# One kernel, one edit: all score tiles of a head pair before its value products, in attention run beside a feed-forward layer

## What is computed

```python
scores = 1.0 / np.sqrt(64) * np.matmul(q, k.transpose(0, 1, 3, 2))
scores = cap * np.tanh(scores / cap)
scores = scores - np.max(scores, axis=-1, keepdims=True)
attn = np.exp(scores)
attn = attn / (np.sum(attn, axis=-1, keepdims=True) + 1e-09)
x = np.matmul(attn, v)                 # then (B*S, H*D) = (1792, 768)
r = np.maximum(x @ w_in, 0.0)
y = (s * (r * r) + b) @ w_out
```

## Time and profile before

| | us |
|---|---|
| median of three runs | 625.81 |
| lowest, highest | 625.52, 625.81 |
| the profiled execution's own time | 625.56 |
| its span, from first to last instruction | 623.8 |

### The profile page before, as it was taken

One profiled execution on the slowest core, in us unless ns is written; L12 is line 12 of the kernel. 1 busy time (PEld: TensorE's weight loads), 2 busy tenths in 40 slices (PEclk: granted clock), 3 DMA queues, 4 the chain that ended last, 5 costly groups with the idle time before them and its releaser, 6 DMA issues.

```text
span 623.8 us, 8172 instructions
## 1 busy us (share of the span) xinstructions
PE 617.9 (99%) x3206; PEld 480.8 (77%) x3206; DVE 331.4 (53%) x565; ACT 258.3 (41%) x272; POOL 46.0 (7%) x46
## 2 busy tenths in 40 slices
PE   8999999999999999999999999999999999999998
PEld 4335666777777777777779999999988888888998
DVE  5986999998677677677663332222411121111221
ACT  7985455656555555555413322222411121111220
POOL 0115724700000000000000000000000000000000
PEclk9999999999999999999999999999999999999999
DMA  8432245342222222221014111222522234111501
GB/s 293 139 118 61 87 155 158 107 132 92 73 92 87 76 88 91 71 92 58 29 60 145 62 51 55 73 73 80 172 78 59 68 106 130 48 38 31 171 2 64
DMA packets 31863, 57.17 MB, mean 92 GB/s; under 512 B 3536, under 2 KB 18000, under 8 KB 31824
## 3 DMA queue, kind: packets, MB, share of 16 engines
q1 hardware_dynamic: 31824, 56.64, 28.0%
HBM read 40.11 MB, written 16.52 MB: 91 GB/s over the span
## 4 chain that ended last, share of the span: by engine, by line
PE 96%; ACT 2%; DVE 1%; issue 1%; DVEq 0%; ACTq 0%
PE banks L480 13%; PE banks L482 13%; PE banks L481 13%; PE banks L493 12%; PE banks L492 12%; PE banks L494 12%; PE banks L438 8%; PE banks L393 5%; PE banks L352 3%; PE banks L450 2%; PE banks L418 1%; ACT e L636 1%; PE banks L461 1%; PE banks L509 0%; ACT e L623 0%
## 5 line engine op out<-in xcount | busy, mean ns | idle before, releaser
L480 PE MATMUL banks<-x_hi,w_hi 128*128 128x448 f32 x384 | 142.9, 372 | 0.0
L482 PE MATMUL banks<-x_hi,w_lo 128*128 128x448 f32 x384 | 140.7, 366 | 0.0
L481 PE MATMUL banks<-x_lo,w_hi 128*128 128x448 f32 x384 | 140.6, 366 | 0.0
L493 PE MATMUL banks<-x_lo,w_hi 128*128 128x512 f32 (+2 forms) x384 | 139.4, 363 | 0.0
L494 PE MATMUL banks<-x_hi,w_lo 128*128 128x512 f32 (+2 forms) x384 | 139.4, 363 | 0.0
L492 PE MATMUL banks<-x_hi,w_hi 128*128 128x512 f32 (+2 forms) x384 | 139.4, 363 | 0.0
L821 DVE SCALAR_TENSOR_TENSOR x_lo<-e,beside,x_hi 128x512 fp32r<-128x512 f32 (+1 forms) x48 | 32.5, 684 | 115.4 <-ACT x_hi L650 115.4
L480 PEld LDWEIGHTS banks<-x_hi,w_hi 128*128 128x128 f32 x384 | 72.1, 188 | 15.0 <-issue 8.3
L650 ACT ACTIVATE x_hi<-e,beside 128x512 fp32r<-128x512 f32 (+1 forms) x48 | 31.7, 669 | 116.7 <-PE banks L494 116.7
L492 PEld LDWEIGHTS banks<-x_hi,w_hi 128*128 128x128 f32 x384 | 72.1, 188 | 9.0
L493 PEld LDWEIGHTS banks<-x_lo,w_hi 128*128 128x128 f32 x384 | 72.1, 188 | 8.9
(11 more groups left out here) (67 smaller groups left out, 551.3 us busy)
## 6 DMA issues: line engine op xcount, KB each, us to landing
hidden_scratch<-hidden_sb SPq DMA_DIRECT2D x48, 224.0 KB, 1.9
beside<-q_k SPq DMA_DIRECT2D x23, 448.0 KB, 3.9
e<-hidden_scratch SPq DMA_DIRECT2D x32, 256.0 KB, 2.7
e<-w_out SPq DMA_DIRECT2D x16, 384.0 KB, 3.0
work<-w_in SPq DMA_DIRECT2D x22, 256.0 KB, 5.5
v_sb<-v SPq DMA_DIRECT2D x24, 192.0 KB, 2.5
y_t<-beside SPq DMA_DIRECT2D x10, 256.0 KB, 2.1
e<-hidden_scratch SPq DMA_DIRECT2D x16, 160.0 KB, 2.2
```

Source lines behind the costliest of these rows:

```text
L480: nc.tensor.matmul(out, w_hi[:, j, w], x_hi[:, batch % 2, c, :], start=c == 0, stop=False)
L481: nc.tensor.matmul(out, w_hi[:, j, w], x_lo[:, batch % 2, c, :], start=False, stop=False)
L482: last = nc.tensor.matmul(out, w_lo[:, j, w], x_hi[:, batch % 2, c, :], start=False, stop=c == CT - 1)
L493: nc.tensor.matmul(out, w_hi[:, j, w], ring(x_lo, n), start=False, stop=False)
```

## The change

1. In slots 6 to 22, tile 2 of pair p+1 (A2 B2) is computed right behind tiles 0 and 1, ahead of `values(p)`. It goes to the two `hid` banks. Two waits stand for that: `free_hidden` (before tile 2: the hidden tiles of the slot before have been rectified) and one in `hidden_chunk` (before the first hidden tile of a slot: `last_tanh` has read tile 2). The wait ahead of the next pair's scores is now on `first_read` and, for an odd pair, on the new semaphore `tails_read`.
2. The tail scores go to banks 2 and 3, and ACT reads them with a tanh of their own (`tails_tanh`), so an even pair has two instructions of 128x896 where it had one of 128x1792.
3. A slot's share is whole hidden tiles: 2, 2, 3, 2, 2, 3 in slots 6 to 11 and 3, 2, 3, 3, 2, 3 in each later batch (`tiles_beside`). The number of matmuls is the same.
4. On ACT `first_tanh` and `last_tanh` stand together at the front of the slot, and `split_high` behind them.
5. In `invert`, the copies to `quads` are sums over one element, and the reciprocal is taken four times, straight into `recips`, where one reciprocal and four copies stood.
6. On DVE the first tile of a slot is squared before `invert` and the others behind it.

The diff, with most of its context and two like hunks left out:

```diff
--- before.py
+++ after.py
@@ -33,10 +33,12 @@
 PIECES = CT * FF // PIECE
-CHUNKS = JT * CT
-SHARE = CHUNKS // PAIRS
-EARLY = 2 * CT
+EARLY = 2
+FIRST_ENDS = (4, 6, 9, 11, 13, 16)
+ENDS = (3, 5, 8, 11, 13, 16)
+assert len(ENDS) == len(FIRST_ENDS) == PAIRS and ENDS[-1] == FIRST_ENDS[-1] == JT
@@ -194,16 +197,19 @@
-        def chunks_of(batch, c):
-            if batch == 0:
-                share = (CHUNKS - EARLY) // PAIRS
-                return EARLY + share * c, EARLY + share * (c + 1)
-            return SHARE * c, SHARE * (c + 1)
-        def tiles_in(first, last):
-            return [j for j in range(JT) if first <= CT * j + CT - 1 < last]
+        def tails_group(p):
+            return (p - PAIRS) // 2
+        def tiles_beside(batch, c):
+            ends = FIRST_ENDS if batch == 0 else ENDS
+            first = EARLY if batch == 0 else 0
+            return range(ends[c - 1] if c else first, ends[c])
+        def first_tiles(batch):
+            return [tiles_beside(batch, c).start for c in range(PAIRS) if (batch + 1) * PAIRS + c + 1 < ALL] if batch < B - 1 else []
@@ -313,9 +319,9 @@
                 if p == PAIRS:
-                    for j in tiles_in(0, EARLY):
+                    for j in range(EARLY):
                         store_hidden(j)
-                for j in tiles_in(*chunks_of(batch - 1, c)):
+                for j in tiles_beside(batch - 1, c):
                     store_hidden((batch - 1) * JT + j)
@@ -352,6 +358,19 @@
+            def free_scores(p):
+                pe.wait_ge(first_read, first_group(p - 1))
+                if p == PAIRS + 1:
+                    pe.wait_ge(last_read, last_group(PAIRS))
+                elif p % 2:
+                    pe.wait_ge(tails_read, tails_group(p - 1))
+            def free_hidden(p):
+                batch, c = divmod(p - 1, PAIRS)
+                pe.wait_ge(relu_done, (batch - 1) * JT + tiles_beside(batch - 1, c).start)
             def first_scores(p):
@@ -360,7 +379,7 @@
-                if p > 0:
+                if 0 < p <= PAIRS:
                     pe.wait_ge(first_read, first_group(p - 1))
@@ -370,7 +389,7 @@
                 else:
-                    pe.wait_ge(last_read, last_group(p - 1))
+                    free_scores(p)
                     for t in range(FULL - 1):
@@ -470,6 +488,9 @@
                     pe.wait_ge(last_read, last_group(PAIRS - 1))
+                if c == 0 and j in first_tiles(batch):
+                    pe.wait_ge(last_read, last_group((batch + 1) * PAIRS + first_tiles(batch).index(j) + 1))
                 if batch == 0 and c == 0 and j % JPP == 0:
@@ -539,24 +560,24 @@
                 if p + 1 < SPLIT:
                     first_scores(p + 1)
+                    free_hidden(p + 1)
+                    last_scores(p + 1, G1)
                 elif p + 1 < ALL:
                     first_split_scores(p + 1)
+                    free_hidden(p + 1)
+                    last_split_scores(p + 1, G1)
                 values(p)
...
                     tail_values(p - 1, 2)
-                if p + 1 < ALL:
-                    pe.wait_ge(first_read, first_group(p + 1))
-                    if p % 2:
-                        tail_scores((p + 1) // 2, 0)
-                    bank = 2 if p % 2 else 0
-                    if p + 1 < SPLIT:
-                        last_scores(p + 1, bank)
-                    else:
-                        last_split_scores(p + 1, bank)
-                for chunk in range(*chunks_of(batch - 1, c)):
-                    hidden_chunk(batch - 1, chunk)
+                    if p + 1 < ALL:
+                        pe.wait_ge(first_read, first_group(p + 1))
+                        tail_scores((p + 1) // 2, 2)
+                for j in tiles_beside(batch - 1, c):
+                    for c_in in range(CT):
+                        hidden_chunk(batch - 1, CT * j + c_in)
@@ -604,6 +625,12 @@
                 act.wait_ge(last_done, p + 1)
+                if p > PAIRS:
+                    tile = tile_of(p, FULL - 1, 0)
+                    nc.scalar.activation(e[:, tile:tile + 2, :], hid[:, :, 0:S], ACT.Tanh, scale=tanh_scale
+                                         ).then_inc(last_read, 1)
+                    return
                 if p % 2 == 0:
@@ -619,8 +646,16 @@
                 else:
-                    source = banks[:, 0:2, 0:S] if p % 2 else banks[:, 0:4, 0:S]
+                    source = scores[:, :, 0:S]
                 nc.scalar.activation(e[:, group_of(p, 1), :], source, ACT.Tanh, scale=tanh_scale).then_inc(last_read, 1)
+            def tails_tanh(p):
+                act.wait_ge(tails_done, p // 2 + 1)
+                act.wait_ge(pv_done, products(p - 1))
+                act.wait_ge(e_sum_done, 3 * p)
+                nc.scalar.activation(e[:, G1:G1 + 2, :], scores[:, 2:G1, 0:S], ACT.Tanh, scale=tanh_scale
+                                     ).then_inc(tails_read, 1)
@@ -633,6 +668,8 @@
                 act.wait_ge(last_read if group else first_read, last_group(p) if group else first_group(p))
+                if group and p > PAIRS and p % 2 == 0:
+                    act.wait_ge(tails_read, tails_group(p))
                 nc.scalar.activation(e[:, group_of(p, group), :], e[:, group_of(p, group), :], ACT.Exp, scale=cap_c
@@ -667,20 +704,21 @@
                 exponential(p, 1)
-            for j in tiles_in(0, EARLY):
+            for j in range(EARLY):
                 rectify(j)
...
                 batch, c = divmod(p, PAIRS)
-                if SPLIT <= p + 2 < ALL:
-                    split_high(p + 2)
                 if p + 1 < ALL:
                     first_tanh(p + 1)
+                    last_tanh(p + 1)
+                    if SPLIT <= p + 2 < ALL:
+                        split_high(p + 2)
                     exponential(p + 1, 0)
-                if p + 1 < ALL:
-                    last_tanh(p + 1)
+                    if p % 2:
+                        tails_tanh(p + 1)
                     exponential(p + 1, 1)
-                for j in tiles_in(*chunks_of(batch - 1, c)):
+                for j in tiles_beside(batch - 1, c):
                     rectify((batch - 1) * JT + j)
@@ -760,18 +798,17 @@
                 for k in range(1, P // BLOCK):
-                    nc.vector.tensor_copy(quads[:, k, :], parts[k * BLOCK:(k + 1) * BLOCK, :]).then_inc(quads_done, 1)
+                    nc.vector.tensor_reduce(quads[:, k, :], parts[k * BLOCK:(k + 1) * BLOCK, :].unsqueeze(2), AX.X, ALU.add
+                                            ).then_inc(quads_done, 1)
                 dve.wait_ge(quads_done, P // BLOCK * (m + 1))
-                nc.vector.tensor_reduce(totals[:, 0, :], quads[:].rearrange("p k n -> p n k"), AX.X, ALU.add
+                nc.vector.tensor_reduce(totals[:], quads[:].rearrange("p k n -> p n k"), AX.X, ALU.add
                                         ).then_inc(totals_done, 1)
                 dve.wait_ge(totals_done, m + 1)
-                nc.vector.reciprocal(totals[:, 1, :], totals[:, 0, :]).then_inc(inverse_done, 1)
-                dve.wait_ge(inverse_done, 2 * PAIRS + m + 1)
...
                     head = k * BLOCK // D
-                    nc.vector.tensor_copy(recips[k * BLOCK:(k + 1) * BLOCK, 0, :],
-                                          totals[:, 1, head * BLOCKS:(head + 1) * BLOCKS]).then_inc(spread_done, 1)
+                    nc.vector.reciprocal(recips[k * BLOCK:(k + 1) * BLOCK, 0, :],
+                                         totals[:, head * BLOCKS:(head + 1) * BLOCKS]).then_inc(spread_done, 1)
                 dve.wait_ge(spread_done, P // BLOCK * (m + 1))
@@ -878,12 +915,11 @@
                     add_last_e(p + 1)
-                start, end = chunks_of(batch - 1, c)
-                for j in tiles_in(start, start + 8):
-                    square((batch - 1) * JT + j)
+                tiles = tiles_beside(batch - 1, c)
+                square((batch - 1) * JT + tiles[0])
                 if p + 1 < ALL:
                     invert(p + 1)
-                for j in tiles_in(start + 8, end):
+                for j in tiles[1:]:
                     square((batch - 1) * JT + j)
             for j in range(JT):
```

More of the change, by code:

```diff
@@ L92, in attention_ffn @@
         quads = sb("quads", [BLOCK, P // BLOCK, 2 * BLOCKS], F32)
-        totals = sb("totals", [BLOCK, 2, 2 * BLOCKS], F32)
+        totals = sb("totals", [BLOCK, 2 * BLOCKS], F32)
         r_sum = sb("r_sum", [P, 2, S], F32)
@@ L141, in attention_ffn @@
         last_read = sem("last_read")
+        tails_read = sem("tails_read")
         exp_done = sem("exp_done")
```

## The result

| | before | after |
|---|---|---|
| median, lowest to highest (six runs each, same chip), us | 625.66, 625.38 to 625.82 | 621.49, 621.08 to 621.78 |
| the profiled execution's own time, us | 625.56 | 621.75 |
| its span, us | 623.8 | 619.7 |

The ratio is 0.9934, 95% interval 0.9921 to 0.9947: 4.2 us faster, where 3.1 were foreseen (622.7, range 621.3 to 624.5).

What follows compares the result with a forecast made beforehand. TensorE's own work was taken as the bound. Joined score runs save 0.6 us (slots 6 to 8) plus 2.5 (9 to 22), 3.1 in all: 625.56 to 622.4, median 622.7 us; range 621.3 to 624.5.

Steps and rivals of the forecast that it cites:

- What bounds the kernel: TensorE, busy 99% of the span, waits for nobody from slot 6; only its own work or new waits move time.
- Edges, 3.1 us: Joining two score runs into one saves 0.20 us in each of slots 6 to 8, 0.18 in 9 to 22.
- The seam that is left: Hidden matmuls straight behind values (even slots) or tail scores (odd): no extra cost, values staying 2.41 us, tail scores 0.86.
- Rival (a): The seam moves and only half the edge is saved in 17 slots: 1.5 us, 624.3 us; chance 0.12.
- free_hidden: TensorE's new wait before tile 2 for the previous slot's last hidden tile to be rectified: margin 0.5 us, cost zero.
- Tile 2's tanh: First hidden tile waits until ACT has read tile 2: margin 0.12 us in seven even slots, 10 to 22.
- or the cast ahead of them: With the cast ahead of the two tanh on ACT, the margin of the first hidden tile's wait would be missed.
- worth nothing by itself: Cheaper invert saves DVE about 2 us beside POOL, but off the path, since TensorE doesn't wait for DVE.
- Whole tiles at zero: Shares of whole hidden tiles: same chunk count, some slots shorter, some longer, last slot ending at the same matmul; no gain counted.
- Rival (c): Late cast, DVE can't catch up in slots 8 to 11, late stores hold rectify and TensorE: 628.1 us; chance 0.05.
- rival (b): Hidden matmuls' pace changes: slots 12 to 22 faster, 620.8 us, chance 0.05; or slots 6 to 11 slower, 623.6, 0.03.
- the same pace as before: Sign that the forecast is right: hidden matmuls keep their pace, 0.203 us in slot 7 and 0.2065 in slot 14.

Runs made afterwards that it cites:

- seam_more: Changed kernel with tile 2 computed between the first and second value tiles, two more runs in each of 17 slots: 626.83 us, ratio 1.0015 to the kernel before.
- exp_between: Changed kernel with ACT's first exponential put between the tanh of tiles 0 and 1 and that of tile 2: 636.25 us, ratio 1.0172 to the kernel before.
- cast_first: Changed kernel with the cast of q and k (split_high) back at the front of ACT's slot: 621.06 us, ratio 0.9929 to the kernel before.
- old_invert: Changed kernel with the old copies back in invert: 622.05 us, ratio 0.9942 to the kernel before.
- whole_tiles: Kernel before with only the shares made whole hidden tiles, old invert kept: 629.7 us, ratio 1.0052 to the kernel before.
- cast_first_old_invert: Changed kernel with both the cast back at the front of ACT's slot and the old copies in invert: 624.08 us, ratio 0.9975 to the kernel before.

## Why the prediction was right

By its own steps:

- **What bounds the kernel**: held. TensorE has no wait from slot 6 on, and all of the gain is its own work.
- **Edges, 3.1 us**: measured 3.30. The 0.18 a run, read off rows in which two tiles and one tile stand apart, is also the mean of 34 further runs in seam_more.
- **The seam that is left, taken at zero**: held, 2.41 and 0.86 to the next start, now with hidden matmuls behind them. Rival (a), 624.3, falls.
- **`free_hidden`**: no wait in the kernel after. **Tile 2's tanh**: margin 0.2 for 0.12; the order of the two tanh is worth the 15 us that exp_between lost.
- **"or the cast ahead of them"** (it would be missed): wrong, and by the prediction's own numbers. It had the cast's end at T + 1.47 and `first_tanh`'s start at T + 1.53, so the cast fits ahead of it. cast_first shows it.
- **`invert` "worth nothing by itself"**: wrong. It was read from TensorE's waits before, where the slots were long enough. With the shorter whole-tile slots DVE is late in slots 9 to 11, and the new `invert` is what covers it: 1.45 us of the stretch in the one profiled execution of old_invert (0.6 of the median, not clear of noise), 3.2 us of the median in the order of before. The new `invert` in the kernel before, with its old shares, wasn't run. The 2 us per `invert` beside POOL was 2.8.
- **Whole tiles at zero**: it fits the sum only with the new `invert`; alone they were 4 us slower, and with the new `invert`, in the order of before, 0.9. Rival (c) had this chain, a late load, late DVE, stores on SP, but feared the cast's new place; that place covers the late load, and the danger lay in the shares with the old `invert`.
- **Pace**: rival (b), with 0.05 on the faster side, came in part: there are 330 slow matmuls fewer than 528, net 1.25 us of its 1.9. The forecast's sign "the same pace as before" didn't hold. This is the term that the sum left out and most of the surplus. The range left this rival's full size, 620.8, out. The measured 621.49 is 0.2 above the range's lower end because 330 matmuls changed and not 528, which nothing in the prediction foresaw; that part is luck.

The balance of the spans: 3.12 foreseen for the edges, + 0.18 there, + 1.25 of pace, - 0.51 of a late start that repeats of either kernel show to be chance, is 4.04 of 4.1.

## What to carry to other kernels

Where TensorE is the bound, count its runs of unlike tiles: each run here cost 0.15 to 0.20 us, and joining two gained that in each of 17 slots, since the wait for the bank was hidden by another run. When a step is called free since nobody waits for it, ask whether the same change shortens what covers it: take it out of the changed kernel, not only of the old one. And measure a kernel's repeated matmuls slot by slot, since equal ones may not be equally fast.

## What the hardware showed that I had not expected

Equal hidden matmuls (128 by 128, 448 columns, each with its weight load) keep one of two paces for a whole run of 36 to 54, 202.7 or 206.7 ns. The same slots were slow in both executions of the same kernel, with stretches equal to a nanosecond over 254 us. In kernels without a wait of TensorE in the stretch the choice follows the order and lengths of the runs ahead, and a new table of shares moved those at 206.7 ns from 360 to 36. A wait changes it: the same queue on TensorE had 198 slow matmuls without a wait, and 54, 144 and 252 with some.

A wait of 1.92 us of TensorE (whole_tiles) was followed by a granted clock of 0.60 on average over 4 us and another 1.5 us lost, and one of 1.78 (cast_first_old_invert, 7 us behind one of 0.53) by 0.57 from 137 to 141 us. Waits of 1.40 (old_invert) and up to 1.65 (exp_between) were not: the granted clock stayed at 1.00.
